# Moving two waits, one register load and one elementwise operation in a fused attention and mixture-of-experts kernel

## The reference

```python
# 1. gated linear attention: B, H, S, D = 2, 8, 768, 40, step by step over S
m_new = maximum(f + m, i);  f_stab = exp(f + m - m_new);  i_stab = exp(i - m_new)
C = f_stab * C + i_stab * outer(v, k);  n = f_stab * n + i_stab * k
y[t] = sigmoid(o) * (C @ q) / maximum(abs(n @ q), 1)
# 2. x: 1536 tokens x 320. Mixture of 8 experts, two for each token
noisy = x @ w_gate + log1p(exp(x @ w_noise)) * noise      # the top 2, softmax over both
out[token] += weight * (relu(x[token] @ w1[e]) @ w2[e])   # 320 -> 1024 -> 320
# 3. a second mixture: 4 experts, every token through all of them
out += p[:, e] * (relu(x @ w1[e]) @ w2[e])                # p: probabilities, normed
```

## Time and profile before

| | us |
|---|---|
| median of 3 runs | 701.12 (700.65 to 703.75) |
| the profiled execution | 700.65 |
| its span in the trace | 698.5 |
| PE busy | 683.6 (98% of the span) |
| DVE busy | 389.6 (56%) |
| ACT busy | 288.1 (41%) |
| POOL busy | 104.2 (15%) |

### The profile page before, as it was taken

The page is one execution under the profiler, slowest core; times in us unless marked ns, Lnnn a source line. Parts: engine busy times, 40 slices in busy tenths (PEclk is TensorE's granted clock), DMA queues, the critical chain, the costliest instruction groups (busy, mean ns, idle before and its releaser), DMA issues.

```text
span 698.5 us, 11335 instructions
## 1 busy us (share of the span) xinstructions
PE 683.6 (98%) x4297; PEld 625.5 (90%) x4297; DVE 389.6 (56%) x656; ACT 288.1 (41%) x494; POOL 104.2 (15%) x145
## 2 busy tenths in 40 slices
PE   9999999999999999999899999999999999999996
PEld 7999976999999999999789988988898898898986
DVE  6687854766655754654565455545546545454432
ACT  5545534555443643543443243433424333242311
POOL 7433202522022020023311002012000001000000
PEclk9999999999999999999999999999999999999999
DMA  7447641755544748911752433435224143341001
GB/s 227 119 120 201 205 154 38 240 169 152 165 146 122 210 142 299 340 61 54 233 181 78 123 90 114 136 108 165 85 81 132 63 135 114 90 129 38 0 0 38
DMA packets 28810, 92.52 MB, mean 132 GB/s; under 512 B 4672, under 2 KB 10816, under 8 KB 28768
## 3 DMA queue, kind: packets, MB, share of 16 engines
q1 hardware_dynamic: 21472, 76.22, 35.7%
q0 software_dynamic: 3072, 10.49, 5.2%
q10 hardware_dynamic: 4224, 5.24, 2.1%
HBM read 76.87 MB, written 15.07 MB: 132 GB/s over the span
## 4 chain that ended last, share of the span: by engine, by line
PE 95%; DVE 1%; ACT 1%; issue 1%; DMA 1%; POOL 0%; DVEq 0%; ACTq 0%; POOLq 0%
PE pY L1356 13%; PE pY L1358 13%; PE pY L1357 13%; PE pH L1341 10%; PE pH L1342 10%; PE pH L1343 10%; PE pH L1348 5%; PE pH L1346 5%; PE psYa L1228 3%; PE pH L1292 2%; PE psD L1143 2%; PE psS L1163 2%; PE psYa L1248 1%; PE pT L1318 1%; PE psL L1271 1%
## 5 line engine op out<-in xcount | busy, mean ns | idle before, releaser
L648 ACT ACTIVATE h_hi<-pH 128x512 fp32r<-128x512 f32 x160 | 95.7, 598 | 276.2 <-PE pH L1348 271.9
L1023 DVE SCALAR_TENSOR_TENSOR h_lo<-pH,h_hi 128x512 fp32r<-128x512 f32 x160 | 110.5, 691 | 163.8 <-ACT h_hi L648 160.2
L1356 PE MATMUL pY<-w_hi,h_hi 128*128 128x320 f32 x608 | 189.0, 311 | 1.9 <-DVE h_lo L1023 0.7
L1358 PE MATMUL pY<-w_hi,h_lo 128*128 128x320 f32 x608 | 187.5, 308 | 0.0
L1357 PE MATMUL pY<-w_lo,h_hi 128*128 128x320 f32 x608 | 187.4, 308 | 0.0
L1341 PE MATMUL pH<-x_hi,w_hi 128*128 128x512 f32 (+3 forms) x324 | 122.9, 379 | 1.4 <-issue 0.9
L788 DVE TENSOR_TENSOR w_lo<-stage,w_hi 128x1024 fp32r<-128x1024 f32 (+1 forms) x80 | 108.5, 1358 | 26.3 <-ACT w_hi L575 26.1
L1356 PEld LDWEIGHTS pY<-w_hi,h_hi 128*128 128x128 f32 x608 | 114.1, 188 | 10.0 <-issue 5.5
L1342 PE MATMUL pH<-x_lo,w_hi 128*128 128x512 f32 (+3 forms) x324 | 120.4, 372 | 0.0
L1343 PE MATMUL pH<-x_hi,w_lo 128*128 128x512 f32 (+3 forms) x324 | 119.9, 370 | 0.0
L1357 PEld LDWEIGHTS pY<-w_lo,h_hi 128*128 128x128 f32 x608 | 114.1, 188 | 3.3
(11 more groups left out here) (265 smaller groups left out, 650.1 us busy)
## 6 DMA issues: line engine op xcount, KB each, us to landing
stage<-in_w SPq DMA_DIRECT2D x40, 640.0 KB, 4.0
stage<-in_w SPq DMA_DIRECT2D x40, 512.0 KB, 3.5
stage<-in_w SPq DMA_DIRECT2D x40, 256.0 KB
results_by_slot<-X SPq DMA_DIRECT2D x9, 640.0 KB, 8.7
results_by_slot<-acc ACTq DMA_DIRECT2D x8, 640.0 KB, 3.3
qk<-in_qk_t SPq DMA_DIRECT2D x16, 240.0 KB
kv<-in_kv_n SPq DMA_DIRECT2D x8, 480.0 KB
og<-in_o_n SPq DMA_DIRECT2D x2, 960.0 KB, 6.4
```

The costliest lines, as they stand in the source:

```text
L648: act.activation(HH[s % 2][:, :], pH[s % 2][:, :], ACT.Relu).then_inc(hh_done[layer], 1)
L1023: dve.scalar_tensor_tensor(out=HL[s % 2][:, :], in0=pH[s % 2][:, :], scalar=0.0, in1=f32(HH[s % 2][:, :]), op0=ALU.max, op1=ALU.subtract). ...
L1356: pe.matmul(y[:, 0:XD], hh, wh, start=(f == 0), stop=False)
L1358: return pe.matmul(y[:, 0:XD], hl, wh, start=False, stop=(f == NF - 1))
```

## The change

Four things are moved. SP's wait ahead of layer 2's loads is for `gathered[1][1]` and not for `layer1_mm`. In attention, the gate operation of a pair follows the `outputs` of the same pair, with its wait for `o_ready` ahead of these, and no longer stands before the `outputs` of the next. DVE waits for `layer1_mm` ahead of the mixing of the four near tiles and not behind it. PE loads the count `used` behind the 32 selection matmuls and not ahead of them. No operation is added or taken away.

```diff
--- before.py
+++ after.py
@@ -396,7 +396,7 @@
             def load_second(w, u):
                 load_weights(1, E1 + u, lambda n: w * PIECES + n + 1)
 
-            sp.wait_ge(layer1_mm, 1)
+            sp.wait_ge(gathered[1][1], 32)
             for u in range(1, E2):
                 load_second(u, u)
             with sp.Fori(1, BLOCKS) as b:
@@ -823,10 +823,6 @@
                 dve.reciprocal(rden[:, :, :], rr[:, :, :]).then_inc(y_chain, 1)
                 dve.wait_ge(y_chain, 4 * i + 3)
                 dve.tensor_tensor(yt[:, :, :, :], Ya[:, :, :, 0:D], rden[:, :, :].unsqueeze(3).to_broadcast([P, CH, 2, D]), ALU.mult).then_inc(y_read, 1)
-
-            def gated(i):
-                if i * B % PAIRS == 0:
-                    dve.wait_ge(o_ready, i * B // PAIRS + 1)
                 dve.wait_ge(y_read, i + 1)
                 xo = X[:, :, :].rearrange("p (c b) n -> p c (b n)", b=B)[:, :, i * 2 * D:(i + 1) * 2 * D]
                 dve.scalar_tensor_tensor(out=xo, in0=og[:, i, :, :, :].rearrange("p c h d -> p c (h d)"), scalar=1.0,
@@ -841,10 +837,9 @@
                 carried(i, par)
                 mults(i, 1, par)
                 states(i, par)
-                if i >= 1:
-                    gated(i - 1)
+                if i * B % PAIRS == 0:
+                    dve.wait_ge(o_ready, i * B // PAIRS + 1)
                 outputs(i)
-            gated(PAIRS - 1)
             dve.wait_ge(y_chain, 4 * PAIRS)
             dve.sem_inc(x_done, 1)
 
@@ -1080,6 +1075,7 @@
             dve.sem_inc(wl_done[1], 2 * PIECES)
             dve.wait_ge(hl_done[0], STEPS * used + H_CREDIT)
             dve.sem_inc(hl_done[1], H_CREDIT)
+            dve.wait_ge(layer1_mm, 1)
             for tt in range(BT):
                 near_1, near_2 = (t[:, tt % 2, :] for t in near_G[tt // 2])
                 dve.wait_ge(last_out, tt + 1)
@@ -1087,7 +1083,6 @@
                 dve.scalar_tensor_tensor(out=near_1, in0=near_1, scalar=w_rest[:, 0, tt:tt + 1], in1=XB[:, tt, :], op0=ALU.mult, op1=ALU.add).then_inc(mix, 1)
                 dve.wait_ge(mix, tt + 1)
                 dve.scalar_tensor_tensor(out=XB[:, tt, :], in0=near_2, scalar=w_rest[:, 1, tt:tt + 1], in1=near_1, op0=ALU.mult, op1=ALU.add).then_inc(x2_ready, 1)
-            dve.wait_ge(layer1_mm, 1)
             for half in range(2):
                 c = slice(half * HALF, (half + 1) * HALF)
                 for k in range(3):
@@ -1416,8 +1411,6 @@
             with pe.Fori(0, MUST // 2) as j:
                 for q in range(2):
                     visit_by_count(2 * j + q, j, q, (lengths >> (MUST - 1 - q - 2 * j)) & 1, j < MUST // 2 - 1 if q else None)
-            pe.wait_ge(rt_tiles, 2)
-            used = pe.value_load(counts[0:1, 0:1], min_val=MUST, max_val=V1)
             pe.wait_ge(sel_made, ST)
             for tt in range(BT):
                 for n in range(ST):
@@ -1427,6 +1420,8 @@
                             pe.wait_ge((yh_done, yl_done)[m], n + 1)
                         ins = pe.matmul(last_bank[tt][:, 0:XD], sel_t[r, n, tt * P:(tt + 1) * P], y[r, :], start=(n + m == 0), stop=(n + m == ST))
                 ins.then_inc(last_mm, 1)
+            pe.wait_ge(rt_tiles, 2)
+            used = pe.value_load(counts[0:1, 0:1], min_val=MUST, max_val=V1)
             with pe.If(used > MUST):
                 pe.wait_ge(last_out, BT)
                 pe.wait_ge(y_copied[1], 2 * MUST + COPY_CREDIT)
```

## The result

The changed kernel takes 710.15 us (median of 3 runs, 709.64 to 713.24), the kernel before 701.12. The ratio is 1.0131, with a 95% interval of 1.0096 to 1.0167: slower by 9.0 us, and outside the forecast range of 703.6 to 708.4. The fifteen executions of the changed kernel on record reach from 707.96 to 713.69. The profiled one has a span of 707.8 us against 698.5, and in the chain that ended last, read from the page, PE has lost four points of the 95 that it held in the earlier trace rows.

The account below looks back on a forecast made before the run. PE's stream, 95% of the chain that ended last, was taken as the bound. Terms 1.75 + 2.46 + 0.47 + 0 = 4.7 us took the profiled 700.65 to 705.3; with 0.47 for the median, 705.8 us, range 703.6 to 708.4.

Parts of the forecast that it names:

- The fourth term: SP's queue of weight loads: expert 1's six loads go out about 5.4 us sooner; 0, bounds -0.3 and +3.6.
- The third: PE's register load, moved ahead of the branch at the joint, delays layer1_mm by 0.47 us; bounds 0 and 0.8.
- The rival's own reckoning: PE's branch at the joint: early loads delay its code and double its length, +3.6 us to 709.4; chance 0.09.
- The argument against it: Against early loads slowing PE's branch: the 640 KB store of results was in flight beside it too.
- DVE's wait: Joint of layers 1 and 2: mixing starts after layer1_mm, layer 2's first matmul +2.46 us; bounds 1.8 and 3.9.
- The gate: Attention: moved gate delays the next pair's product of half 0; 7 x 0.25 = 1.75 us, bounds 0 and 2.7.
- 0.04 us for the reader's latency: Attention: product's end to PE's reading, taken from the first pair, making PE 0.25 us later a pair.
- The bound of 0.39 a pair: Attention: PE's lateness a pair if the 0.18 us between product and reader is all latency; 7 x 0.39 = 2.7.
- The clock rival: Joint: PE's granted clock falls to 0.50 in the longer hole, adding 1.7 us, to 707.5; chance 0.26.
- the rule weighed there: PE's clock: low is the default, activity lifts it, and transposes do not count as busy in the same way.
- The slack rival: Attention, L1228: slack swallows the product's lateness, so the gate's 1.75 us becomes 0; 704.0, chance 0.15.
- The figure of the Trainium skill weighed in the forecast: PE's branch at the joint: a compare-and-branch takes about 108 ns; the forecast used the measured 3.56 us instead.

Follow-up runs that it names:

- e1: Kernel before with SP's wait alone changed, to gathered[1][1]; 704.17 us, ratio 1.0046.
- e5: Changed kernel with SP's wait put back to layer1_mm; gate, DVE's wait and register load stay moved; 708.18 us, ratio 1.0093.
- e7: Kernel before with ACT's store of the last visit's results issued behind the fourth weighing, not the second; 700.59 us, ratio 0.9999.
- e4: Kernel before with PE's register load alone moved behind the selection matmuls; 703.30 us, ratio 1.0027.
- e10: Changed kernel with SP's wait put back and PE's block for spare visits left out with its branch; 703.85 us, ratio 1.0054.
- e9: Kernel before with the gate operation put behind the next pair's product of half 0, ahead of qg; 703.01 us, ratio 1.0022.
- e3: Kernel before with DVE's wait for layer1_mm alone moved ahead of the mixing; 703.07 us, ratio 1.0013.
- e12: Changed kernel again, unaltered, for a second profile; 710.69 us, ratio 1.0147 against the kernel before.
- e2: Kernel before with the gate operation of attention moved alone; 704.16 us, ratio 1.0051.
- e8: Kernel before, unchanged, for a second profile; 700.51 us, ratio 0.9987.
- e6: Kernel before with SP's wait changed and PE's block for spare visits left out with its branch; 704.30 us, ratio 1.0046.
- e11: Kernel before with three filler matmuls of 512 columns ahead of PE's selection matmuls; 700.92 us, ratio 0.9995.

## Why the prediction was wrong

**The step that failed is the branch's length, taken to be as long as before whatever was moved around it.** It entered the sum twice. The fourth term, SP's wait, was put at 0; alone (e1) it measured 3.1 us, and on top of the other three the branch goes from 5.08 us (e5) to 6.86, which brings `layer1_mm` another 1.7 us later. The third, the register load, was put at 0.47 and measured 2.3 (below). The forecast saw that the loads would go out at 332.3 and share the DMA engines with "whatever PE's sequencer fetches in its long branch", and gave this 0.09. That is what happened. The rival's own reckoning, 709.4 us, was 0.8 short of the measured time; that is close in part by luck, since of the 3.3 us by which the branch grew, 1.5 came with the moved register load (5.08 in e5) and not with the loads. The argument against it, that the store had been in flight too, left out which came first. The earlier trace rows have the branch's start at 333.9, and the store's issue stands behind it:

```profile
334.08 0.38 ACTq L653 DMA_DIRECT2D results_by_slot<-acc  x1
```

What matters is who is first in the queue, and e7 has the same branch with no store in flight when it begins.

**The register load** (0.47) was nearly right in its own length, 0.6 to 0.8 us of later start, and missed what it lets past: the store goes ahead of the code (e4, 5.08 us). In e5, at full clock, the branch ends 3.0 us behind the start of the last selection matmul (342.68 against 339.7), and 0.66 before: 2.3 us. This term, too, is the queue's.

**DVE's wait** (2.46): the mixing and the splits took the forecast course. From the start of mixing to the first matmul the changed kernel needs 5.97 us against 5.48 worked out. At full clock (e10) it is 5.72: the sum was 0.24 short, because the third split waits for ACT's copy (L722), and the low clock adds 0.25 by holding PE in its transposes. By e10 the whole term hangs on the branch: without it, it is 0. This term and the branch's aren't independent costs to be added, as the forecast put them; the wait turns every microsecond of the branch into one of the joint, and without it (e1) ACT's copies, behind the same semaphore, do it.

**The gate** (1.75) measured 2.8. The step that failed is the choice of 0.04 us for the reader's latency; the row had 0.18, and 0.15 is what the hole shows. (The first pair of the changed kernel has 0.04 again; why it differs is open.) The bound of 0.39 a pair is met by the 0.40 measured, but in part by luck: the product comes 0.48 later and not 0.39, as the gate's extra 0.09 us beside POOL's mask wasn't foreseen. e9 adds that the chain behind the product would have given nearly the same by itself.

**The clock rival** (0.26) happened besides the others, not in their stead: the five profiles in which `layer1_mm` leaves PE a hole at full clock (the changed kernel, e1, e3, e5, e12) all have it there; of the others, e2, e4, e8 and e9 had fallen earlier, at 332.7 to 336.4 us, e6 falls later, at 348.1, and the kernel before, e7, e10 and e11 stay at full clock through the joint. It cost 0.25 us up to the first matmul and 0.7 behind it in the profiled execution. Of the rule weighed there (the Trainium skill, "TensorE: Matmul & The Clock Gate", "Part 4: PE-mode transpose"), this trace agrees so far as PE's clock stays at 0.50 through 3.6 us of transposes, 346.8 to 350.4, with PE busy 0.93 to 1.00 of each whole microsecond in them.

**The slack rival** (0.15) is refuted by the hole at L1223.

**The branch's price.** PE has other branches, and those are cheap: the twelve of L1385 in the kernel before take 67 to 210 ns. The figure of the Trainium skill weighed in the forecast ("Advanced Engine Details and Errata", "Control Flow Timing") fits these and none of the twelve over the spare visits, of which 3.46 us is the shortest. The Trainium skill, "Advanced Engine Details and Errata", "ISA Cache", says that a sequencer keeps its code in lines of 16 KB, or 256 instructions; the one packet of 16 KB behind each of these branches agrees.

**By times:** SP's wait lies between e5 (1.0093) and the changed kernel (1.0131 and, again, 1.0147), whose intervals overlap a little, so that here the traces decide: `layer1_mm` comes 3.1 us behind the start of the last selection matmul in e5 and 4.8 and 4.9 in the two profiles of the changed kernel. Between e5 and e10 (1.0093 against 1.0054) lies the branch behind the moved load, with DVE's wait and the clock. e10 and e2 (1.0054 and 1.0051) leave the gate.

**Why the branch is 3.5 us in some executions and 3.9 to 4.2 in others** (e2, e3, e9) the packet of code tells. Its own time, its share of 16 engines over 0.2 us, is 1.07 us in e7, 1.26 before, 1.49 in e2 and 1.80 in e3, beside the store; in e9 it takes 1.20 but begins 1.35 us behind the branch and not 1.0. From the packet's end to the branch's end it is 1.2 to 1.5 us in all twelve profiles, and 1.4 in most.

## What to carry to other kernels

Before a transfer is released earlier, look at what else goes to the DMA engines in the next ten microseconds: besides data, an engine's own code behind a long taken branch, and a store that somebody waits for. A wait on a semaphore that another engine raises behind such a branch inherits the branch's length; wait on the data itself where that suffices. An operation of an engine that is level with the bound belongs in its idle gap, and a measured gap between writer and reader is to be read as latency until a row shows otherwise.

## What the runs showed of the hardware

- PE's taken branch over the unexecuted block lasted 3.46 us with the DMA queues empty (e7), 3.5 to 4.2 with a 640 KB store issued just behind it, 5.08 with that store ahead of it (e4, e5), and 6.4 to 6.9 with loads ahead of it, 1.6 of 2.9 MB in the changed kernel. The 16 KB packet of code began 1.0 us after the branch's start at the least and 4.5 at the most, and the branch ended 2.3 to 3.2 us behind the packet's start, 1.2 to 1.5 behind its end.
- Code, the store from ACT's queue and the loads from SP's went through the DMA engines nearly in the order of issue: the code began after 1.56 of the 1.57 MB issued ahead of it in the changed kernel, and after 527 and 526 of the store's 528 packets in e4 and e5; in e1 it began after 1.25 MB.
- PE's sequencer raised a semaphore written behind the matmuls up to 2.7 us before the last of them started (e6, 334.1 against 336.85).
- In five of eight pairs a VectorE operation of 0.66 us took 0.75 beside a GpSimd mask, and the mask 1.16 us instead of 0.86; in the first pair the operation kept its 0.66 and the mask took 1.21.
- PE's clock falls to half at 18 to 22, 92 to 95, 121 to 124 or, at the joint, in 332 to 353 us in some executions and not in others of the same or nearly the same kernel. From one profile each, such a stretch is worth 1.3 us at 92 and 4.9 at the joint (e8: 253.7 us from the first L1356 to the first L1119, against 248.8 before), as much as any single part of this change.
